# Scores prepared ahead are spread over four tiles instead of three, and the row work of tiles one and two is moved

## The reference

```python
# attention, per batch and head
q_d, k_d, v_d = means of q, k, v over 4 positions each          # 144 positions
out_up    = repeat(softmax(q_d k_d^T / 8) v_d, 4)
out_local = softmax(where(|i - j| < 4, q k^T / 8, -1e9)) v      # 7 keys for a query
x = (out_up + out_local) laid out as tokens x 512
# layer 1                       # layer 2
h = x @ w_in                    h = x @ w_in2
x = (h * sigmoid(h)) @ w_out    x = (s * relu(h)**2 + b) @ w_out2
```

## Time and profile before

| what | value |
|---|---|
| median of 3 runs | 943.24 us (943.19 to 943.6) |
| the profiled execution | 941.09 us, its span 939.3 us, mean granted clock 0.996 |
| PE busy | 923.6 us, 98% of the span |
| PEld / DVE / ACT / POOL busy | 852.5 / 438.8 / 372.5 / 459.9 us |
| DMA | 68.75 MB, mean 73 GB/s |
| tiles of layer 1 start at | 112.60 (t = 1), 184.50, 251.72, 312.94 us (t = 4) |

### The profile page before, as it was taken

How to read it: one execution, slowest core, us unless ns; L and a number is a source line. 1 busy time by engine, 2 the same in 40 slices (tenths; PEclk the granted TensorE clock), 3 DMA queues, 4 the chain that set the end, 5 groups by cost and what they waited for, 6 DMA issues and landing times.

```text
span 939.3 us, 15644 instructions
## 1 busy us (share of the span) xinstructions
PE 923.6 (98%) x5975; PEld 852.5 (91%) x5975; DVE 438.8 (47%) x909; ACT 372.5 (40%) x999; POOL 459.9 (49%) x444
## 2 busy tenths in 40 slices
PE   8999999799999999999999999999999999999998
PEld 8899999799999999999999988888888888888897
DVE  5577536647556466574655642233224222322232
ACT  5666443434544545435345632232224222322332
POOL 6677557959778688685652222213222222222222
PEclk9999999999999999999999999999999999999999
DMA  6655363343342522522006530011002000100000
GB/s 171 194 149 174 80 152 87 86 113 83 89 109 64 133 69 60 147 62 61 25 22 218 158 104 1 1 54 37 0 1 89 0 0 0 67 0 0 33 13 23
DMA packets 87170, 68.75 MB, mean 73 GB/s; under 512 B 38720, under 2 KB 73024, under 8 KB 87104
## 3 DMA queue, kind: packets, MB, share of 16 engines
q1 hardware_dynamic: 87104, 67.86, 26.6%
HBM read 52.76 MB, written 15.08 MB: 72 GB/s over the span
## 4 chain that ended last, share of the span: by engine, by line
PE 87%; DVE 4%; ACT 3%; POOL 3%; issue 1%; DMA 1%; SPq 0%; ACTq 0%; POOLq 0%; DVEq 0%
PE pH L815 21%; PE pY L830 21%; PE pH L758 17%; PE pY L763 16%; PE pS L593 3%; PE pS L596 1%; PE pO L657 1%; DVE w_in_hl L319 1%; POOL weighted L1521 1%; PE pO L643 1%; PE pO L619 1%; DVE w_out_hl L319 1%; POOL g_hl L319 1%; ACT w_in_hl L854 1%; POOL x_hl L319 1%
## 5 line engine op out<-in xcount | busy, mean ns | idle before, releaser
L319 POOL TENSOR_TENSOR g_hl<-act,g_hl 128x288 fp32r<-128x288 f32 (+2 forms) x208 | 200.5, 964 | 443.7 <-ACT g_hl L854 443.3
L763 PE MATMUL pY<-g_hl,w_out_hl 128*128 128x288 f32 x1536 | 236.9, 298 | 2.5 <-POOL g_hl L319 2.5
L758 PE MATMUL pH<-x_hl,w_in_hl 128*128 128x288 f32 x1518 | 230.4, 299 | 4.4 <-POOL x_hl L319 3.2
L758 PEld LDWEIGHTS pH<-x_hl,w_in_hl 128*128 128x128 f32 x1518 | 210.6, 189 | 5.4 <-issue 4.3
L763 PEld LDWEIGHTS pY<-g_hl,w_out_hl 128*128 128x128 f32 x1536 | 212.0, 188 | 3.4 <-POOL g_hl L319 3.4
L815 PE MATMUL pH<-x_hl,w_in_hl 128*128 128x512 f32 (+1 forms) x960 | 208.4, 368 | 0.0
L830 PE MATMUL pY<-w_out_hl,g_hl 128*128 128x512 f32 x864 | 207.8, 390 | 0.0
L815 PEld LDWEIGHTS pH<-x_hl,w_in_hl 128*128 128x128 f32 x960 | 169.0, 188 | 31.0
L830 PEld LDWEIGHTS pY<-w_out_hl,g_hl 128*128 128x128 f32 x864 | 161.3, 188 | 33.1 <-POOL g_hl L319 0.3
L1408 DVE TENSOR_TENSOR act<-act 128x512 f32<-128x512 f32 (+1 forms) x80 | 55.5, 694 | 270.6 <-ACT act L1091 270.6
L854 ACT ACTIVATE g_hl<-act 128x288 fp32r<-128x288 f32 (+2 forms) x208 | 103.9, 500 | 191.0 <-DVE act L1410 103.8
(11 more groups left out here) (141 smaller groups left out, 759.5 us busy)
## 6 DMA issues: line engine op xcount, KB each, us to landing
qk_f<-qk SPq DMA_DIRECT2D x32, 292.0 KB, 3.3
vd_f<-vp SPq DMA_DIRECT2D x64, 144.0 KB
stage_in<-w_in SPq DMA_DIRECT2D x32, 256.0 KB, 2.9
stage_out<-w_out SPq DMA_DIRECT2D x32, 256.0 KB, 2.9
v_loc<-vp SPq DMA_DIRECT2D x24, 240.0 KB, 5.0
score_bands<-act SPq DMA_DIRECT2D x48, 114.8 KB, 2.4
qk_f<-qk SPq DMA_DIRECT2D x64, 72.0 KB, 2.7
x_scratch<-y_sb SPq DMA_DIRECT2D x8, 576.0 KB, 3.7
```

The lines of the kernel that those rows point to most:

```text
L319: eng.tensor_tensor(lo, full, hi.bitcast(F32), ALU.subtract).then_inc(signal, 1)
L758: last = pe.matmul(pH[:, f % 2, 0:T1], w_in[:, wp, c, f * P:(f + 1) * P], x1[:, par, mp, c, :], start=c + n == 0, stop=c == C - 1 and n == 2)
L763: last = pe.matmul(pY[:, c, 0:T1], w_out[:, wp, f, c * P:(c + 1) * P], g_hl[:, f % RING, mp, 0:T1], start=f + n == 0, stop=f == NF - 1 and ...
```

## The change

Tile 0 takes unit 16's turning and unit 17's scores into its last slot. Tile one visits heads 2 to 11, tile two 4 to 12, tile three 5 to 14 (before: 1 to 12, 5 to 14, 7 to 14). The two slots in front with two visits start with an even head, and some slots, the last ones of tiles one and two among them, have no visit. The row softmax of tiles one and two goes to the end of a slot (`SOFTMAX_LAST`), the products, sums and turns go with it, and ACT takes a visit's exponents before it copies the attended heads.

```diff
-UNITS_IN = {1: [(1, 2), (3, 4), (5, 6), (7, 8), (9,), (10,), (11,), (12,)],
-            2: [(5, 6), (7, 8), (9,), (10,), (11,), (12,), (13,), (14,)]}
-SOFTMAX, SOFTMAX_IN = 1, {1: 4, 2: 2}
+UNITS_IN = {1: [(2, 3), (4, 5), (6, 7), (8, 9), (), (10,), (11,), ()],
+            2: [(4, 5), (6, 7), (8,), (9,), (10,), (11,), (12,), ()],
+            3: [(5, 6), (7, 8), (9,), (10,), (11,), (12,), (13,), (14,)]}
+SOFTMAX, SOFTMAX_IN, SOFTMAX_LAST = 1, {1: 3, 2: 2, 3: 2}, (1, 2)
-WEIGH_IN = {1: {4: ((), (0,)), 5: ((1, 2), (3,)), 6: ((4, 5), (6,)), 7: ((7, 8), ())},
-            2: {2: ((), (0,)), 3: ((1,), (2,)), 4: ((3,), (4,)), 5: ((5,), (6,)), 6: ((7, 8), ())}}
+WEIGH_IN = {1: {4: ((0,), (1,)), 5: ((2, 3), (4,)), 6: ((5, 6), (7, 8))},
+            2: {3: ((0,), (1,)), 4: ((2,), (3,)), 5: ((4,), (5,)), 6: ((6,), (7,)), 7: ((8,), ())},
+            3: {2: ((), (0,)), 3: ((1,), (2,)), 4: ((3,), (4,)), 5: ((5,), (6,)), 6: ((7, 8), ())}}
-SUM_IN = {1: {5: ((0,), (1, 2), ()), 6: ((3,), (4, 5), ()), 7: ((6,), (7, 8), ())},
-          2: {3: ((0,), (1,), ()), 4: ((2,), (3,), ()), 5: ((4,), (5,), ()), 6: ((6,), (7,), (8,))}}
+SUM_IN = {1: {4: ((), (0,), (1,)), 5: ((), (2, 3), (4,)), 6: ((), (5, 6), (7, 8))},
+          2: {3: ((), (0,), (1,)), 4: ((), (2,), (3,)), 5: ((), (4,), (5,)), 6: ((), (6,), (7,)), 7: ((8,), (), ())},
+          3: {3: ((0,), (1,), ()), 4: ((2,), (3,), ()), 5: ((4,), (5,), ()), 6: ((6,), (7,), (8,))}}
-TURNS_IN = {1: {(6, 36): 0, (7, 2): 1, (7, 47): 2}, 2: {(5, 36): 0, (6, 36): 1, (7, 12): 2}}
-ONE_UNIT, LAST_UNIT, FIRST_LAST_UNIT, TWO_UNITS = 15, 24, 20, (7, 31)
+TURNS_IN = {1: {(5, 36): 0, (6, 36): 1, (7, 22): 2}, 2: {(4, 36): 0, (6, 36): 1, (7, 20): 2},
+            3: {(5, 36): 0, (6, 36): 1, (7, 12): 2}}
+ONE_UNIT, LAST_UNIT, TWO_UNITS, TWO_UNITS_IN = 15, 24, (7, 31), {1: (10, 34)}
+QK_SUMS_AT = {(1, 4): 12, (1, 6): None}
+V_SUMS_AT = {(1, 5): None, (1, 7): 10, (2, 6): None, (2, 7): 12}
-TRANS_AT, SCORES_AT, ATTEND_AT, LAST_ATTEND_AT = 9, 15, 38, 34
+TRANS_AT, SCORES_AT, ATTEND_AT = 9, 15, 38
+LAST_TRANS_AT, LAST_SCORES_AT, LAST_ATTEND_AT, NEXT_AT = 3, 7, 20, 34
...
+        def qk_pair(t, u):
+            now = units(t, u)
+            if (t, u) in QK_SUMS_AT:
+                return QK_SUMS_AT[t, u]
+            return now[-1] + now[-1] % 2 if now and (len(now) == 2 or now[0] % 2) else None
+        def v_pair(t, u):
+            now, before = units(t, u), units(t, u - 1) if u else ()
+            if (t, u) in V_SUMS_AT:
+                return V_SUMS_AT[t, u]
+            if now and now[0] % 2 == 0:
+                return now[0]
+            return before[1] if len(before) == 2 and before[1] % 2 == 0 else None
...  SP, tile 0
                     store_band(unit(h, H))
+                    store_band(unit(h, H + 1))
+                    read_band(unit(h, H))
+                    load_qk(unit(h, H + 4))
+                    load_v(unit(h, H + 2))
                     sp.wait_ge(win_ready, NF)
                     sp.wait_ge(wout_ready, NF)
                     load_windows((2, 0, 1))
+                def ask(h, k):
+                    if w := unit(h, k + 3):
+                        load_qk(w)
+                    if w := unit(h, k + 1):
+                        load_v(w)
...  SP, tile1; `last` is set in the last slot with a visit, if its head is odd
+                            if len(now) == 2:
+                                if w := unit(h, k):
+                                    store_band(w)
+                                if k < H and (w := unit(h, k - 1)):
+                                    read_band(w)
+                                if k == H - 1:
+                                    read_band(unit(h, k))
+                                if k % 2:
+                                    ask(h, k)
+                                if k > H and (w := unit(h, k - 1)):
+                                    read_band(w)
+                                continue
...
+                        if last:
+                            ask(h, now[-1])
...  PE, tile 0, in small()
+                    if k == NEXT_AT and last:
+                        trans_unit(unit(h, H))
+                        score_unit(unit(h, H + 1))
...  ACT, a visit (visit() was pooled())
                     if w := unit(h, v - 1):
                         pT_copy(w)
+                    if w := unit(h, v):
+                        exps(w)
                     for n in (v - 3, v - 2):
                         if v % 2 and (w := unit(h, n)):
                             evacuate(w)
...  ACT at the end of slot_rows; DVE has row_shift there and row_normalise at the next slot's start
+                    if softmax_last(t, u):
+                        row_exps(t, h)
+                    if alone:
+                        place(t, h, here[0])
                         for c in range(C):
                             x_round(t, h, c)
...  DVE, end of slot_rows
+                    if softmax_last(t, u):
+                        row_shift(t, h)
                     for i in sums[2]:
                         sum_row(t, i)
-                    if late(t, u):
+                    if alone:
                         for c in range(C):
                             x_add(t, h, c)
...  ends of tile0: ACT, DVE, POOL
+                    visit(prepared(1), 1)
+                    maxima(unit(h, H + 1))
+                    normalise(unit(h, H + 1))
+                    qk_sums(unit(h, H + 2))
...  POOL, slot_rows
+                    if qk_now and len(now) != 1:
+                        qk_sums(qk_now)
+                    if v_now and now and now[0] % 2 and not finish:
+                        v_sums(v_now)
                     for i in first:
                         weigh(t, i)
...
                     g_low(L[0], t, UPS[u][0], T1)
+                    if qk_now and len(now) == 1:
+                        qk_sums(qk_now)
+                    if v_now and not finish and not (now and now[0] % 2):
+                        v_sums(v_now)
...
                     for i in second:
                         weigh(t, i)
                     for f in UPS[u][1:]:
                         g_low(L[0], t, f, T1)
-                    if late(t, u):
+                    if alone:
                         for c in range(C):
                             x_low(t, h, c)
```

More of the change, by code:

```diff
@@ L372, in groups, with last_alone, softmax_last, places @@
             return [g for (slot, k), g in turns(t).items() if slot == u]
-        def late(t, u):
-            return t == 1 and u == H - 1
+        def last_alone(t, u):
+            return u == H - 1 and not units(t, u)
+        def softmax_last(t, u):
+            return t in SOFTMAX_LAST and u == softmax_in(t)
+        def places(t, u):
+            now = units(t, u)
+            if len(now) == 2:
+                return TWO_UNITS_IN.get(t, TWO_UNITS)
+            return (ONE_UNIT if u < H - 1 else LAST_UNIT,)[:len(now)]
+        def visited(t, u, k):
+            before = [v for s in range(u + 1) for v, at in zip(units(t, s), places(t, s)) if (s, at) < (u, k)]
+            return before[-1] if before else units(t, 0)[0] - 1
+        def qk_pair(t, u):
+            now = units(t, u)
+            if (t, u) in QK_SUMS_AT:
[8 more added lines that the diff above has]
+            return before[1] if len(before) == 2 and before[1] % 2 == 0 else None
         with nc.Block() as block:
@@ L1001, in slot_rows @@
                     two = len(now) == 2
-                    finish = u == H - 1 and not late(t, u)
+                    alone = last_alone(t, u)
+                    finish = u == H - 1 and not alone
                     if u == 1:
@@ L1005, in slot_rows @@
                         g_high(L[0], t, CARRIED, 2, T1)
-                    if u == H - 1:
+                    if finish:
                         place(t, h, here[0])
@@ L1014, in slot_rows @@
                     if two:
-                        pooled(h, now[0])
-                        exps(unit(h, now[0]))
+                        visit(h, now[0])
                     g_high(L[0], t, f, 2, T1)
-                    if u == softmax_in(t) != SOFTMAX:
+                    if u == softmax_in(t) != SOFTMAX and not softmax_last(t, u):
                         row_exps(t, h)
@@ L1022, in slot_rows @@
                             x_round(t, h, c)
-                    if not two:
-                        pooled(h, now[0])
-                        if w := unit(h, now[0]):
-                            exps(w)
+                    if len(now) == 1:
+                        visit(h, now[0])
                     if u < H - 1:
@@ L1327, in slot_rows @@
                             x_add(t, h, c)
-                    if not two and (w := unit(h, now[0])):
+                    if len(now) == 1 and (w := unit(h, now[0])):
                         maxima(w)
-                    if u == softmax != SOFTMAX:
+                    if u == softmax != SOFTMAX and not softmax_last(t, u):
```

(26 more changed lines are left out.)

60 lines of the change are left out of this document (26 added, 34 removed).

## The result

| | before | changed kernel |
|---|---|---|
| median of the runs | 943.24 us (942.92 to 943.99, 5 runs) | 955.23 us (951.22 to 956.44, 5 runs) |
| profiled execution | 941.09 (span 939.3, clock 0.996) | 951.22 (span 949.4, clock 0.998) |

The ratio is 1.012 (95% interval 1.0103 to 1.0136). I had predicted 947.9, with 952.0 as the upper end: the sign was right, the size 7.3 us too small. The profiled execution is the fastest of the changed kernel's five; the other four have a mean clock of 0.993 to 0.995 and are 3.0 to 5.2 us longer.

A forecast was written before the change was run, and what follows sets the result against it. PE, busy 98% of the span, was taken as the bound, its work unchanged. New waits of 14.8 us less 10.1 gave +4.7 on 941.09, so 945.8, and 2.15 for the median gave 947.9; 8-in-10 range 938.5 to 952.

The forecast's parts named there:

- down 0 and head 3's turning: Start of tile 1: PE waits 0.7 us for POOL, then 2.2 for the copy behind band 18's landing.
- double slots "lose nothing more": Tile 1's slots with two visits: no further wait, as probabilities come half a microsecond earlier; 0 us.
- down 9 and turn 0: Tile 1: PE waits 1.3 us at down 9 for POOL and 1.9 at turn 0 for sum 2.
- turn 2 and tile 2's start: End of tile 1: PE waits 1.1 us at turn 2, then 2.0 in all for the `x_low` pieces.
- turns 0 and 2 of tile 2, tile 3's start: PE waits 1.0 us at turn 0, 2.4 at turn 2 for sum 8, and 1.5 at tile 3's start.
- tile 3's last slot: Tile 3 inherits tile 2's old last slot; 0.7 us of new waits.
- The empty last slot: Rival: at the ends of tiles 1 and 2 it pays, new waits some 2.5 us, total 935.6; chance 0.22.
- The last step of tile 2's `row_shift`: Moved behind gate 6 into an idle stretch of POOL, it costs 0.4 us; 2.0 us gained.
- product 0 of tile 1: First product of tile 1's rows: starts at 158.0 us, when POOL is through with pair 28's `qk_sums`.
- The third rival: New waits also bring PE's clock down, each fall 1.7 us, total 949.6 to 951.3; chance 0.17.
- all upper bounds at once: All new waits of tiles 1 to 3 at their upper bounds: 20.9 us, so +10.8, 954 us.

The follow-up runs named there:

- a2: Changed kernel with the four window loads of tile 1's rows issued behind band 18's store and its read; 950.11 us, ratio 1.0065 to before.
- a3: Changed kernel with POOL taking pair 28's sums in slot 7 of tile 1, behind the products; 950.81 us, ratio 1.0083 to before.
- a6: a1, a2 and a3 together on the changed kernel, value sums behind `x_low`, pair 26 loaded before band 23's read, tile 2's products a slot sooner; 937.64 us.
- a1: Changed kernel with POOL taking `g_low` 0 ahead of pair 20's sums in slot 0 of tile 1; 953.20 us, ratio 1.0105 to before.

## Why the prediction was right in sign and wrong in size

The sum was made for profiled executions: +4.7, and it came out at +10.1. Tile 0 took 69.08 us instead of the 70.4 of the forecast, because its first slot took 7.4 us and not 8.8: before, the granted clock over 42 to 52 was 0.83, here 1.00. That is 1.3 in the change's favour that it had not earned: luck. After tile 4's start both kernels take the same to 0.3. So tiles 1 to 3 are 6.9 over the forecast:

| step of the prediction | forecast | measured |
|---|---|---|
| down 0 and head 3's turning (slots 0 and 1 over 8.7 each) | 0.7 + 2.2 | 4.95 |
| double slots "lose nothing more" (slots 2 and 3, block down 7) | 0 | 0.67 + 0.6 |
| down 9 and turn 0 (slot 5) | 1.3 + 1.9 | 4.9 |
| turn 2 and tile 2's start | 1.1 + 2.0 | 3.6 |
| turns 0 and 2 of tile 2, tile 3's start | 1.0 + 2.4 + 1.5 | 6.3 (1.8 + 2.3 + 2.2) |
| tile 3's last slot | 0.7 | 0.7 |

- **What was right.** All ten waits came where the prediction put them, behind the releasers it named, and beside them only two small ones (0.49, 0.37): POOL before down 0, a landing ahead of head 3, pair 28's sums ahead of product 0, sum 2 before turn 0 (1.9 forecast, 1.73 measured), sum 8 before turn 2 of tile 2 (2.4 and 2.29). The empty last slot does not pay by itself. The last step of tile 2's `row_shift` takes 0.29 us (0.4 forecast). Tile 2, though, starts at 189.67 and not between 184 and 187.
- **The step that failed** is the landing of loads and stores on SP's queue, at two places. The first is band 18. I had the mechanism, one copy buffer whose store is queued behind loads, and sized it with a landing 11.7 us after the tile's start; it came 13.7 after. That is the whole 2.0 by which slots 0 and 1 are over. The second is product 0 of tile 1, and there I applied the mechanism too little: band 24's store goes out only behind pair 26's load and lands at 153.9, and pair 28's load, issued behind it, came at 159.8, where I had it in by 156.2. Product 0 so came 9.0 us into slot 4 instead of 6.8, and down 9 and turn 0 lost 4.9 instead of 3.2. a2 and a3 test the two places: 3.0 us of slots 0 and 1, and 2.3 of slot 5. That pair 28's load is late because of band 24's store is read from SP's queue and not tested. In tile 2 product 0 came 5.1 us into slot 3, where I had 3.6 to 4.7: POOL waited 5.51 us for pair 32's values, again a load. Turn 0 there cost 1.8 instead of 1.0; a6, which takes those sums two slots later, has product 0 at 1.9 us and no wait at turn 0. Why tile 3's start cost 2.2 instead of 1.5 stays open.
- **The double slots "lose nothing more"** was wrong in this execution, by 0.67 in slots 2 and 3 and 0.6 at down 7. At 145.48 PE waits 0.49 for head 7, whose copy waited for the store behind the write of `x_scratch`; it landed after 5.0 us. In a1 and a3 the same store landed after 4.5, and slots 2 and 3 took 8.67 to 8.69 each, nothing over their price of 8.7. So the sentence stood on a margin of some tenths, and I had not looked at that store.
- **The two terms at the start of tile 1 were not two.** I added 0.7 and 2.2, and as sizes their sum was 1.8 short of the 4.7 in the timeline. But a1 shows that the first lies inside the second: without it, the second is 4.77. What ends that stretch is one landing.
- **The clock.** The third rival (chance 0.17) came in addition, not in place. In the profiled execution there is one fall, behind the first new wait and not behind tile 2's turn, where I looked for it; by a1 its 1.7 us lie beside the late landing and are no part of the miss. In the four other executions the mean clock is lower (0.993 to 0.995), and the median is 4.0 us above the profiled execution, where I had carried over the 2.15 of before. That is 1.9 of the 7.3. Which waits bring these further falls down no profile here shows.
- **The range** ended at 952, under the 954 of all upper bounds at once, and those bounds were too tight themselves: 20.9 for the new waits, measured 21.7. Slots 0 and 1 cost 4.95 against a bound of 1.4 + 3.0, and the double slots had no bound. None of them allowed for one queue being late at several places, or for a median further above the profiled execution.

The Trainium skill (DMA: Bandwidth & Descriptors, "Queues, rings and completion order") has each DMA engine take a queue's descriptors in ring order. a2 agrees: the same store takes 7.4 us to landing behind the windows and 4.4 ahead of them.

## What to carry to other kernels

Where a buffer is single and its store shares a queue with loads, price every such store in the schedule, not the worst one: here four loads put ahead of one store delayed the next writer of the buffer by 4.9 us (13.8 after the tile's start instead of 8.9). Before adding two waits, ask whether they lie beside the same late event; if they do, the sum is that event's time less PE's work, and removing the first alone brings nothing. And where a change only moves PE's work, order each slower engine's queue anew with it: here the same spread of the scores was 12 us slower, or 5 faster, with the order of the other queues (and the old spread, with part of that order, 2 faster).
